# Clustered attention and two feed-forward layers in fp32 pieces: the first score product of a head moved to the end of its step

## The reference

```python
q_assign = argmax(q_n @ c_n.T);  k_assign = argmax(k_n @ c_n.T)
mask = q_assign[..., :, None] == k_assign[..., None, :]
scores = where(mask, q @ k.T / sqrt(64), -1e9)
attn = exp(scores - max(scores)) / (sum + 1e-9)
x = (attn @ v) as (1536, 512)
h = x @ w_in;   g = P(h) / (Q(h) + 1e-6);   x = g @ w_out
h = x @ w2_in;  g = h - tanh(h);            out = g @ w2_out
```

## Time and profile before

| | |
|---|---|
| median of 3 runs | 801.04 us (800.62 to 801.45) |
| the profiled execution | 804.98 us, its span 803.2 us |
| mean granted TensorE clock | 0.993 |
| busy: TensorE, VectorE, ScalarE, GpSimd | 787.2, 502.9, 503.8, 310.0 us |
| attention stage | step 0 begins at about 21 us, step 95 at 274.6 us |

### The profile page before, as it was taken

The page is one execution under the profiler, slowest core; times in us unless marked ns, Lnnn a source line. Parts: engine busy times, 40 slices in busy tenths (PEclk is TensorE's granted clock), DMA queues, the critical chain, the costliest instruction groups (busy, mean ns, idle before and its releaser), DMA issues.

```text
span 803.2 us, 11576 instructions
## 1 busy us (share of the span) xinstructions
PE 787.2 (98%) x4100; PEld 678.3 (84%) x4100; DVE 502.9 (63%) x777; ACT 503.8 (63%) x964; POOL 310.0 (39%) x346
## 2 busy tenths in 40 slices
PE   8899999999999999999999999999999999999998
PEld 8899999999988777887888888888888888888886
DVE  3788888888878699999877888976211111121111
ACT  4888988988899778888666777767322222222222
POOL 5646566575664342222222222217522222222221
PEclk7999999999999999999999999999999999999999
DMA  5344444334220342000000021125000100010001
GB/s 149 87 118 117 103 123 112 92 100 110 65 74 26 99 132 79 26 1 1 0 1 1 0 80 53 53 75 161 1 0 1 53 0 1 1 41 12 1 1 53
DMA packets 40265, 44.26 MB, mean 55 GB/s; under 512 B 4976, under 2 KB 30480, under 8 KB 40208
## 3 DMA queue, kind: packets, MB, share of 16 engines
q1 hardware_dynamic: 40064, 43.49, 19.4%
q10 hardware_dynamic: 144, 0.03, 0.0%
HBM read 29.40 MB, written 3.19 MB: 41 GB/s over the span
## 4 chain that ended last, share of the span: by engine, by line
PE 81%; DVE 11%; ACT 4%; DMA 1%; SPq 1%; issue 1%; POOL 0%; DVEq 0%; ACTq 0%; POOLq 0%
PE y_ps L1160 27%; PE h_ps L1137 26%; PE s_ps L1066 7%; PE pv_ps L1094 7%; PE pt_ps L1077 7%; PE pr_ps L1027 2%; PE pr_ps L1009 2%; DVE f_a L929 2%; DVE w_lo L890 2%; DVE f_t L935 2%; DVE f_bc L933 2%; DVE f_bc L916 2%; DVE f_t L921 1%; DVE f_t L920 1%; SPq L350 1%
## 5 line engine op out<-in xcount | busy, mean ns | idle before, releaser
L560 POOL TENSOR_TENSOR g_lo<-f_t,g_hi 128x512 fp32r<-128x512 f32 x96 | 125.2, 1304 | 369.0 <-ACT g_hi L668 369.0
L976 DVE TENSOR_TENSOR f_t<-h_ps,f_a 128x512 f32<-128x512 f32 x48 | 33.2, 692 | 203.4 <-ACT f_a L746 203.4
L1137 PE MATMUL h_ps<-x_hi,w_hi 128*128 128x512 f32 x384 | 149.5, 389 | 1.3 <-DVE w_lo L890 1.3
L1137 PE MATMUL h_ps<-x_lo,w_hi 128*128 128x512 f32 x384 | 149.4, 389 | 0.0
L1137 PE MATMUL h_ps<-x_hi,w_lo 128*128 128x512 f32 x384 | 149.4, 389 | 0.0
L668 ACT ACTIVATE g_hi<-f_t 128x512 fp32r<-128x512 f32 x96 | 60.8, 633 | 139.3 <-PE y_ps L1160 123.4
L867 DVE TENSOR_TENSOR pt_lo<-pt_ps,pt_hi 128x384 fp32r<-128x384 f32 x192 | 98.8, 550 | 20.4 <-ACT pt_hi L627 18.8
L627 ACT ACTIVATE pt_hi<-pt_ps 128x384 fp32r<-128x384 f32 x192 | 84.6, 491 | 23.0 <-PE pt_ps L1077 22.2
L854 DVE TENSOR_REDUCE nmax<-s_ps 128x1 f32<-128x768 f32 x96 | 91.1, 949 | 3.9 <-PE s_ps L1066 3.8
L620 ACT ACTIVATE probs<-s_ps,nmax 128x768 f32<-128x768 f32 x96 | 86.8, 905 | 2.8 <-DVE nmax L854 2.7
L1137 PEld LDWEIGHTS h_ps<-x_hi,w_hi 128*128 128x128 f32 x384 | 72.1, 188 | 16.7 <-DVE w_lo L890 1.8
(11 more groups left out here) (137 smaller groups left out, 1523.6 us busy)
## 6 DMA issues: line engine op xcount, KB each, us to landing
w_raw<-in_moe_w_in_dram SPq DMA_DIRECT2D x32, 256.0 KB, 2.8
w_raw<-in_moe_w_out_dram SPq DMA_DIRECT2D x32, 256.0 KB, 3.1
ka<-qk_b SPq DMA_DIRECT2D x32, 192.0 KB, 3.1
raw_q<-in_q_dram SPq DMA_DIRECT2D x16, 192.0 KB, 2.7
raw_k<-in_k_dram SPq DMA_DIRECT2D x16, 192.0 KB, 3.0
raw_v<-in_v_dram SPq DMA_DIRECT2D x16, 192.0 KB, 3.0
qk_b<-qa SPq DMA_DIRECT2D x16, 192.0 KB, 2.6
rz<-z_rows SPq DMA_DIRECT2D x16, 192.0 KB, 3.4
```

The costliest lines, as they stand in the source:

```text
L560: pool.tensor_tensor(g_lo[n % 2][:, :], f_t[n % 2][:, :], g_hi[n % 2][:, :].bitcast(F32), ALU.subtract).then_inc(g_lo_done, 1)
L976: dve.tensor_tensor(f_t[n % 2][:, :], h_ps[n % 4][:, :], f_a[n % 2][:, :], ALU.subtract).then_inc(g_done, 1)
L1137: last = pe.matmul(h_ps[n % 4][:, :], w[f][:, ws], x[:, cols], start=(kt == 0 and i == 0), stop=(kt == KT - 1 and i == 2))
```

## The change

In steps 8, 14, 20, ..., 86 (k at least 6 and k + 4 a multiple of 6) the score product that the step makes is the first of a head, tile k + 4. It no longer stands directly behind `transpose_probs(k)`, but behind the step's early unit (Q1, up to step 74) and its value products. All other steps and all other engines keep their lists. The first products of heads 0 and 1 stay where they are.

```diff
             for k in range(TILES):
                 transpose_probs(k)
                 later = SCORES_AT.get(k, ())
-                for m in later[:1]:
+                in_front = 0 if k >= T and (k + LOOK) % T == 0 else 1
+                for m in later[:in_front]:
                     score_tile(m)
                 for g, u in early_at[k]:
                     unit(g, u)
                 if k >= HT:
                     values(k)
-                for m in later[1:]:
+                for m in later[in_front:]:
                     score_tile(m)
                 for g, u in late_at[k]:
                     unit(g, u)
```

## The result

The changed kernel takes 803.84 us (median of 20 executions, 802.95 to 807.54) and the kernel before 801.17 us (median of 20, 800.06 to 805.24); the ratio is 1.0031, its 95% interval 1.0020 to 1.0043. The forecast was 800.6 with a range to 803.1.

A forecast was written before the change was run, and what follows sets the result against it. TensorE was taken to set the pace; gains of 0.10, 0.36, 0.77 against losses of 0.40, 0.22, 0.20 summed to -0.41 us, giving 804.6 for the profiled execution and 800.6 for the median, range 799.2 to 803.1.

The forecast's parts named there:

- plain heads: Heads where ScalarE does not also copy x_hi; 26, 38, 50, 62 were to lose 0.10 us each, +0.40 in all.
- x heads: Steps 20, 32, 44, 56, 68, 80, where ScalarE also copies x_hi; zero loss forecast for all but 20, which gains.
- the sum of -0.41: Attention stage: all forecast gains and losses of the moved products together, -0.41 us.
- The waits for the one-hot rows: Score products held by hot_t, copied into qk_b; covering them was to give -0.77, -0.36, -0.10 at steps 20, 74, 14.
- T: Start of the transposes of step k; the moved product was to go from T + 0.57 to T + 1.65.
- The 0.87 itself: VectorE: the addition of halves was to start 0.87 us after the row maximum's start.
- Step 8: +0.22: Step 8: three small VectorE instructions between, no idle ahead of the addition, which goes from T + 3.35 to T + 3.57.
- Step 86: +0.20: Step 86, without preparing transposes: the addition was to start at 252.66 instead of 252.46, +0.20 us.
- Slower: Rival, chance 0.15: idle ahead of the addition is no slack, eight plain heads pay 0.44 each; +2.1 us, 803.1.
- The idle 0.26: VectorE's 0.26 us waiting for ScalarE before the addition; was to hide part of the maximum's 0.53 delay, passing on 0.19.
- Faster: Rival, chance 0.13: next values not held by VectorE or ScalarE, TensorE keeps its whole gain of 2.6 us; 798.4.
- about +0.6: Upper bound: each of eight plain heads loses 0.19 us over step 50, while steps 14, 20 and 74 gain.

The follow-up runs named there:

- the second profile: The kernel before profiled once more, with no edit; from step 8 to step 95 it takes 228.3 us, against 230.9 in the changed kernel.

## Why the prediction was wrong

The mechanism in the prediction was right in its form: the product itself costs nothing late, the row maximum comes late, the addition of halves queues behind it, and plain heads pay where x heads are covered. The sign came out wrong because much of the credit was an accident and the debit was undersized. Between the sum of -0.41 and the +2.4 that the pairs show lie 2.8 us: 1.0 is credit for stalls that the second profile doesn't have, 1.1 is the six plain heads (14, 26, 38, 50, 62, 74), 0.57 is step 8 and 0.15 step 86.

- *The waits for the one-hot rows, "-0.77" at step 20, "-0.36" at step 74, "-0.10" at step 14.* The -0.77 is the largest term that failed. I took three stalls of one profiled execution for the kernel's own. The second profile of the same kernel has neither that of step 20 nor that of step 14, only that of step 74; against it the pairs of steps 20, 74 and 14 move by 0, -0.16 and +0.29. Without the -0.77, and with step 14 charged as a plain head, my own sum would have been +0.56 us. I also took the three waits of the earlier trace rows for these three steps. They were these:

```profile
32.29 0.59 PE L1066 MATMUL s_ps<-ka,qa 128*128 128x384 f32 x2 [0.41 <-DMA qk_b<-hot_t]
78.03 0.58 PE L1066 MATMUL s_ps<-ka,qa 128*128 128x384 f32 x2 [0.83 <-DMA qk_b<-hot_t]
218.99 0.59 PE L1066 MATMUL s_ps<-ka,qa 128*128 128x384 f32 x2 [0.21 <-DMA qk_b<-hot_t]
```

  The first is in step 4, at the first product of head 1, which the change leaves where it is; the changed kernel waits 0.4 there too. The others are steps 20 and 74. The delay of 0.2 in step 14 shows only in the start of its scores, T + 0.76 instead of T + 0.57. What makes the rows late at step 20 in some executions stays open. In the first profile the small DMAs landed 3.67 us after the last issue, with the 256 KB weight loads issued behind them, but those are issued at the same place in the executions without a wait.
- *"A plain head therefore loses 0.10."* It lost 0.28. The maximum starts at T + 2.57 instead of T + 2.52, since the nine transposes take 0.90, not 0.855. The hand-over to the addition is 0.99 instead of 0.87. Together the addition is at T + 3.56 instead of T + 3.39. The slack of 0.09 and the latency of 0.15 were right: 156.10 + 0.56 + 0.15 = 156.81.
- *The 0.87 itself.* I read it off pt_lo in front of a maximum and carried it over to a maximum in front of an addition. The Trainium skill (VectorE: DVE Perf Modes, section Two Vector instructions with no wait between them) gives as a model that a Vector instruction whose operand starts in another group of 32 partitions than the last one's in the same memory starts only when all earlier ones have finished. By that rule 0.99 belongs to the plain heads (rows 64 to 127) and 0.87 to the x heads (rows 0 to 63), and the runs agree: 0.99 in the plain heads, where the addition starts 0.03 after the maximum's end shows, and 0.87 in the same heads with rows exchanged and in the uncovered x head. I missed this rule; with it the plain head comes to 0.22.
- *"Step 8: +0.22".* It was +0.79. I moved three small instructions along at their old lengths. In the new place the first meets GpSimd's L487 and takes 0.57. The Trainium skill (Advanced Engine Details and Errata, section VectorE Performance Modes) states that VectorE's second SBUF port is shared with GpSimd, and that GpSimd's instructions and VectorE's two-port ones block each other. The collisions shown here all end within 0.03 us of the end of GpSimd's instruction; whether L962 and L860 ran in a two-port mode no run shows. Another 0.14 lies in step 8, where the Q1 transposes wait for ScalarE's copy of Q0.
- *"Step 86: +0.20".* +0.35. Its addition is on rows 64 to 127 too, and starts 0.99 after its maximum (249.27 to 250.26).
- *"x heads: zero, steps 56 and 57 5.09".* Right to 0.01, for the reason given: without ScalarE's copy they pay. The cover is thin, though: with the late maximum 0.16 of the 0.68 is left.
- *The execution's own time.* I noted that it stood 3.9 us above the median and took that for a constant. It was the low clock of its start, which the stretch at granted clock 0.51 showed.
- *The rivals.* "Slower" had the result's sign and, with 803.1, nearly its size, but by another way: it decided at additions later than T + 3.7, and they came at T + 3.56. The idle 0.26 was real slack: the addition came only 0.36 later, and 0.36 less the 0.09 is the loss. "Faster" fails because TensorE's saving of 0.03 in step 50 is lost in the wait of step 51. The clock stayed at 1.00 in all seven pairs.
- *The bounds.* The upper bound of "about +0.6" does not come out of its own terms: eight times 0.19 less the gains of steps 14, 20 and 74 gives +0.1 to +0.3. It lies below the measured +2.4 either way.

## What to carry to other kernels

When work is moved later on the busiest engine, follow the engine that reads its result: list what queues behind that reader and who waits for it, and look for the latest place at which the reader would not have started anyway. Here that was 0.33 us later (free), and the change went 1.1 us. Before a stall is entered as a gain, it should be in two profiles of the same kernel; and before two executions are compared, their granted clock should be the same.

## What was not expected of the hardware

- Behind a row maximum of 0.95 us the addition of halves starts after 0.87 us or after 0.99 us, by the rows that it works on.
- A VectorE instruction of 4 or 12 elements a row took 0.57 to 0.95 us instead of 0.32 or about 0.2 while a GpSimd instruction with two inputs ran beside it, and ended with it. That the one caused the other is not shown by a run.
- The start-up phase runs at granted clock 1.00 in some executions and partly at the lower level in others (0.51 from 17.2 to 20.5 us). The group at clock 0.994 is 3.2 us slower, and 18 of 73 executions of the kernel before are in it. What decides it was not tried.
